# Attention into experts: side work of the first expert tiles spread over tiles 1 to 6

## The reference

```
f = 1/(1+exp(-f_logit))
state = f[t]*state + outer(k[t], v[t]);  y[t] = q[t] @ state
logits = x @ w_gate + modality_bias[modality_id];  e = argmax(logits)
out[mask] = softmax(logits)[e] * (relu(x[mask] @ w1[e]) @ w2[e])      # experts, F=1024
xn = x/rms(x)*rms_g
y = (silu(xn @ w_gate) * (xn @ w_val)) @ w_out                        # dense layer, F=1536
```

## Time and profile before

| | us |
|---|---|
| runs | 873.43, 869.73, 873.39 (median 873.39) |
| profiled execution, its own time | 871.66 |
| its span in the profile | 869.9 |
| TensorE busy | 835.2 |
| VectorE, ScalarE, GpSimd busy | 470.8, 389.7, 167.0 |
| mean granted clock of TensorE | 0.983 |

### The profile page before, as it was taken

One profiled execution on the slowest core, in us unless ns is written; L12 is line 12 of the kernel. 1 busy time (PEld: TensorE's weight loads), 2 busy tenths in 40 slices (PEclk: granted clock), 3 DMA queues, 4 the chain that ended last, 5 costly groups with the idle time before them and its releaser, 6 DMA issues.

```text
span 869.9 us, 15469 instructions
## 1 busy us (share of the span) xinstructions
PE 835.2 (96%) x5332; PEld 763.1 (88%) x5332; DVE 470.8 (54%) x773; ACT 389.7 (45%) x750; POOL 167.0 (19%) x165
## 2 busy tenths in 40 slices
PE   6999999779999999989999999999999999999997
PEld 6788888779999999989888888888888888888886
DVE  7799998687666666653444343334333333433332
ACT  5788886375666555653322321331242133123112
POOL 5335352408654000000000100110010010001001
PEclk8899999889999999999999999999999999999999
DMA  9767766398988797750200200100020000000000
GB/s 186 159 141 165 172 147 216 139 371 256 294 257 264 245 348 241 267 146 20 73 1 1 73 0 1 64 9 0 0 72 0 0 27 9 0 0 36 0 0 36
DMA packets 44082, 96.49 MB, mean 111 GB/s; under 512 B 9168, under 2 KB 25040, under 8 KB 43920
## 3 DMA queue, kind: packets, MB, share of 16 engines
q1 hardware_dynamic: 39952, 85.81, 33.5%
q0 software_dynamic: 3840, 9.47, 3.0%
q10 hardware_dynamic: 256, 0.79, 0.4%
HBM read 76.75 MB, written 19.29 MB: 110 GB/s over the span
## 4 chain that ended last, share of the span: by engine, by line
PE 77%; issue 1%; DVE 1%; ACT 1%; POOL 0%; DVEq 0%; ACTq 0%
PE h_ps L1778 16%; PE h_ps L1780 15%; PE h_ps L1779 15%; PE ym_ps L1778 7%; PE ym_ps L1780 7%; PE ym_ps L1779 7%; PE xTm_ps L1778 3%; PE xTm_ps L1779 3%; PE xTm_ps L1780 3%; PE xT_ps L1795 1%; PE xTm_ps L1786 1%; POOL out L1442 0%; DVE h_lo L1690 0%; DVE w_lo L1663 0%; ACT w_hi L1460 0%
## 5 line engine op out<-in xcount | busy, mean ns | idle before, releaser
L1753 DVE TENSOR_TENSOR gs<-h_ps,sig 128x512 f32<-128x512 f32 x72 | 49.8, 692 | 178.1 <-ACT sig L1554 178.1
L1554 ACT ACTIVATE sig<-h_ps 128x512 f32<-128x512 f32 x72 | 43.1, 598 | 171.6 <-PE h_ps L1780 171.6
L1565 ACT CAST h_hi<-hid 128x512 fp32r<-128x512 f32 x72 | 44.6, 620 | 150.3 <-DVE hid L1756 150.3
L1778 PE MATMUL h_ps<-x_hi,w_hi 128*128 128x256 f32 x312 | 89.6, 287 | 7.7 <-DVEq L1681 5.1
L1780 PE MATMUL h_ps<-x_lo,w_hi 128*128 128x256 f32 x312 | 89.3, 286 | 0.0
L1779 PE MATMUL h_ps<-x_hi,w_lo 128*128 128x256 f32 x312 | 89.1, 285 | 0.0
L1778 PE MATMUL h_ps<-w_hi,wg_hi 128*128 128x512 f32 x216 | 85.7, 397 | 0.0
L1780 PE MATMUL h_ps<-w_lo,wg_hi 128*128 128x512 f32 x216 | 84.7, 392 | 0.0
L1780 PE MATMUL h_ps<-w_lo,wv_hi 128*128 128x512 f32 x216 | 84.2, 390 | 0.0
L1778 PE MATMUL h_ps<-w_hi,wv_hi 128*128 128x512 f32 x216 | 84.0, 389 | 0.0
L1779 PE MATMUL h_ps<-w_hi,wv_lo 128*128 128x512 f32 x216 | 84.0, 389 | 0.0
(11 more groups left out here) (222 smaller groups left out, 1899.6 us busy)
## 6 DMA issues: line engine op xcount, KB each, us to landing
w_raw<-in_w SPq DMA_DIRECT2D x52, 384.0 KB, 5.1
w_in<-in_w SPq DMA_DIRECT2D x52, 384.0 KB, 5.2
qkf_in<-in_qkf SPq DMA_DIRECT2D x43, 288.0 KB, 4.8
y_sorted<-x_group SPq DMA_DIRECT2D x13, 384.0 KB, 3.4
v_in<-in_v SPq DMA_DIRECT2D x24, 192.0 KB, 4.0
x_regions<-zero_row SPq DMA_DIRECT2D x12, 384.0 KB
x_group<-x_regions SPq DMA_DIRECT2D x12, 384.0 KB, 4.1
g_in<-in_wg SPq DMA_DIRECT2D x3, 768.0 KB, 7.3
```

Of the source, the lines that this page charges most:

```text
L1554: nc.scalar.activation(sig[:], g_ps, ACT.Sigmoid).then_inc(sig_done, 1)
L1565: nc.scalar.copy(h2_hi[:, fb % 2], hid[:]).then_inc(h2_hi_done, 1)
L1753: nc.vector.tensor_tensor(gs[:], g_ps, sig[:], ALU.mult).then_inc(gs_done, 1)
L1778: nc.tensor.matmul(out, hi, rhs_hi, start=first, stop=False)
```

## The change

In the attention's last steps the last tile's keys are no longer turned or copied (they would only feed a state that nobody reads); its reading goes to the bank `ks_ps` that this leaves free, ahead of the rows of the tile before. ScalarE's w1 casts move, and `lo_w1(3)` goes from there into the experts. SyncE loads the first expert's weights ahead of the last two v tiles. In tile 0 ScalarE makes all four w2 casts at once, the count of the last chunk stands in the middle of `hidden(0)`, and the thirds, the scores, exp, table load, token rows and gates leave for the loop: third i to the end of tile i+1, exp and table load to tile 2, token rows to tile 2, gates to tile 3. The by_token writes come 8 each behind thirds 3, 4 and 5; the load of w_out moves from tile 7 to 8.

```
@@ attention, SyncE, then ScalarE
             first.load_weights(sp, e, w1, w2, ahead_sems)
+            for b in range(2):
+                load_v(*tile(CH, b, 2))
-                if t := tile(c, b, 1):
+                if (t := tile(c, b, 1)) and not at(c, CH):      # the copy of turned keys
+                if at(c, CH) and b == 1:
+                    first.hi_w1(nc, act, 3, ahead_sems)
+                    kept(tile(c, b, 2), ks_ps)
...
@@ attention, VectorE and TensorE
-                    first.lo_x(nc, dve, xT_ps, ahead_sems)
-                    first.lo_w1(nc, dve, 3, ahead_sems)
+                if at(c, CH) and b == 2:
+                    first.lo_x(nc, dve, xT_ps, ahead_sems)      # ahead of logits
+                if at(c, CH) and b == 1:
+                    pe.wait_ge(ks_done, NT - 1)
+                    read(c, b, tile(c, b, 2), ks_ps)
...
@@ experts, SyncE
+            for g in range(GR):
+                sp.sem_inc(w2_landed[g], 16)                    # ahead of the two thirds
...
@@ experts, GpSimd
-            pool.wait_ge(pos_ready, 1)
-            pool.wait_ge(gate_ready, 1)
+                if i == KD:
+                    pool.wait_ge(pos_ready, 1)
+                    pool.wait_ge(gate_ready, 1)
...
@@ experts, ScalarE
-            hi_w2(0, 0)
+            for g in range(GR):
+                hi_w2(0, g)
                 hi_h(1)
-                if place == "first":
-                    hi_w2(0, 2)
-                    act.wait_ge(shifted, 1)
-                    nc.scalar.activation(prob, biased, ACT.Exp).then_inc(exp_ready, 1)
-                    nc.scalar.preload_act_table_set("sigmoid_and_others")
-                    hi_w2(0, 3)
...
                 if place == "first":
-                    hi_third(0)
...
-                    with act.If(j < 2 * KD):
-                        for i in range(EARLY, 2 * KD):
-                            with only(act, j, i - 1):
+                    with act.If(j < 2 * KD + 1):
+                        for i in range(2 * KD):
+                            with only(act, j, i + 1):
                                 hi_third(i)
+                                if i == 1:
+                                    act.wait_ge(shifted, 1)
+                                    nc.scalar.activation(prob, biased, ACT.Exp).then_inc(exp_ready, 1)
+                                    nc.scalar.preload_act_table_set("sigmoid_and_others")
@@ experts, VectorE
-            dve.sem_inc(w1_split, GR)
+            dve.sem_inc(w1_split, GR - 1)
             rt.choose(nc, dve, CH - 1, marks, 0)
+            lo_w1(0, GR - 1)
             lo_w2(0, 0)
...
                 if place == "first":
-                    rows_of_tokens()
-                    gates_of_tokens()
+                    rows_of_tiles()
+                if place == "middle":
+                    with dve.If(j < 4):
+                        with only(dve, j, 1):
+                            shifted_scores()
+                        with only(dve, j, 2):
+                            rows_of_tokens()
+                        with only(dve, j, 3):
+                            gates_of_tokens()
```

## The result

Four executions of the changed kernel gave 884.7 to 889.3 us, median 886.88; four of the kernel before 868.9 to 873.43, median 871.56. The ratio is 1.019, with a 95% interval of 1.0165 to 1.0216: slower, inside the range, and 0.9 us from the predicted 886. The profiled execution took 888.39 us (span 886.6), 16.7 us more than that of the kernel before.

The account below looks back on a forecast made before the run. PE, busy 835.2 of 869.9 us, was taken as the bound, so only its stops or slowing count. Terms -0.85, -5.5, +13.8, +1.3 and +5.0 sum to +13.75 us: 885.4 on 871.66, stated as 886, range 878 to 892.

Parts of the forecast that it names:

- end of attention: Barrier between attention and experts: four transposes off the last scatter's chain end it earlier, -0.85 us, bounds nothing and 2.7.
- tiles 0 and 1: First two expert tiles: waits shrink or go and the half clock goes, -5.5 us, bounds 1 and 9.
- waits behind thirds: Loop tiles after thirds 0 to 5: table loads delay `h_lo`, so PE waits before `gather_y(0)`, +13.8 us.
- load in the last tile: Last expert tile: a whole table load ahead of the first square delays `h_hi(0)`, +1.3 us, bounds 0 and 1.3.
- clock: Behind five new PE waits: two in three halve the clock at 1.5 us each, +5.0 us, bounds 0 and 7.5.
- The step that decided: Loop: two loads on ScalarE's chain, less 0.27 us slack, make PE wait 2.5 us behind each of four thirds.
- One sign: Loop turns with two loads: PE waits 2.5 us before `gather_y(0)`, named in the profile as waiting for `h_lo`.
- third 1's tile: Tile after third 1: exp, its table load and the head's load make PE wait 2.8 us.
- rival D: Tiles 0 to 3: early gains fail through a held DVE instruction or late rows and w2; 890 us, chance 0.12.
- A: Loop's table loads: reloading the set already in is nearly free, so not slower; 869.1 us, chance 0.07.
- B: Loop's table loads: they are hidden, leaving only the gains, -6.35 us; 865.3 us, chance 0.04.
- C: Table loads: each costs twice its length since what follows must start afresh; 901 us, chance 0.03.

Follow-up runs that it names:

- after_again: The changed kernel run once more without alteration, on chip C: 885.54 us, ratio 1.0177 to the kernel before.

## Why the prediction was right

The terms of the sum, on the profiled executions:

| term | predicted | measured |
|---|---|---|
| end of attention | -0.85 | -0.74 (163.09 to 162.35; 0.6 from the count on) |
| tiles 0 and 1 | -5.5 | -4.95 |
| waits behind thirds | +13.8 | +15.9 |
| load in the last tile | +1.3 | 0 |
| clock | +5.0 | +6.5 |
| sum | +13.75 | +16.7 |

**The loop.** The step that decided held within 0.06 us in the ordinary tiles: 2.5 us predicted behind thirds 2 to 5, 2.45, 2.45, 2.45 and 2.54 measured; tiles behind no third kept 17.64 us. All of it was read from one chain and a slack of 0.27 us. The loads themselves, 21 in all with the one ahead of attention, each take 1283 ns. One sign came otherwise: these waits are not named as waiting for `h_lo` but as `issue`. In tile 5 `h_lo` ended at 278.59 and PE started at 278.69, so it was `h_lo` all the same.

**The same step failed in one tile.** I put third 1's tile at 2.8 us, of loads and exp. It was 4.96, and 4.95 without any load. I had counted the token rows of VectorE as moved into a tile with room, and not looked at what stands right behind them (`h_lo(0)`) and beside them (GpSimd's split of the third that ScalarE has just cast). The hold on VectorE that I feared elsewhere (rival D) fell on them. ScalarE's relu, behind exp and both loads, ended 1.8 us ahead of the rows (232.65 us), so the later one alone counts:

```profile
230.24 0.60 ACT L1494 ACTIVATE h_hi<-h_ps 128x512 fp32r<-128x512 f32 x1
```

By my estimate from these rows ScalarE alone would have made PE wait 2.7 us, close to the 2.8 predicted. Had I priced the rows at 2.7 us with the 0.60 us of the loop's head, I would have seen 1.9 us even without GpSimd, and hidden behind the loads.

**The end of attention.** VectorE's last instruction ended at 157.71 in place of 160.50, 2.8 us earlier, and GpSimd's last scatter was issued at 157.04 in place of 157.59:

```profile
157.04 0.97 POOL L136 DMA_INDIRECT x_regions<-x_group,row  x1 [0.30 <-issue]
157.53 0.18 DVE L652 TENSOR_REDUCE logits<-x_ps 128x8 f32<-128x32 f32 x1
```

The experts' start moved with the scatter, 0.6 us from the count on, as the step had it. But PE's wait there grew to 5.69 us, where I had written 4.2 as a sign: PE was done with attention 1.4 us earlier and waited for the same scatter.

**Tiles 0 and 1.** The rows of tile 1 were what is late next, as said: 2.54 us at `turn_x`, then 0.84 for `x_lo`. The wait in tile 1 was 0.93 for 0.95 predicted, and no half clock came behind either. The gain was 0.55 us smaller.

**The clock.** Of the waits of 2.45 to 2.54 us one of four was followed by the half level, where I had said two of three. The price was off the other way: behind the wait of 4.96 us the clock stayed at half for 5.6 us, tile 3 lost 25.60 - 17.64 - 4.96 = 3.0 us and tile 4 21.80 - 17.64 - 2.45 = 1.7, and after the loop's exit, where the kernel before had kept its clock, 0.41 of 4.21 us were lost, 1.7. The profile of after_again (885.68 us) has the same waits and half levels in the loop and at its exit, and takes 243.94 us from the experts' first matmul to the exit against 243.84. The 2.7 us between the two executions lie ahead of the experts (159.55 and 162.35), in code that is the same: from 20 to 40 us the granted clock was 1.00 in the one and 0.88 in the other. A difference of 3 us in the total can come from there alone.

```profile
234.04:239.60 5.56, 5.56 (x20) 5.56 (x21) 2.71 (x4) 0.83 (x1) 0.00 (x0) 0.50 0.81 277
278.69:281.70 3.01, 3.01 (x19) 3.01 (x20) 3.01 (x3) 1.76 (x3) 2.62 (x2) 1.00 0.97 284
```

**The last tile.** No wait of 0.25 us stands there, yet the load was not free on ScalarE's side:

```profile
407.23 1.28 ACT L1092 ACT_TABLE_LOAD   x1 [2.42 <-issue]
412.40 0.41 PE L1788 MATMUL ym_ps<-w_hi,h_hi 128*128 128x384 f32 x1 [0.15 <-issue]
```

It began behind the same idle time as the square before, and `h_lo(0)` ended 6.10 us behind the loop's exit in place of 4.78, 1.3 later. PE, at the half clock, was ready for its gather only at 6.06 us behind the exit, 1.5 us later than before. So the whole load that I had counted was there, and hid behind a fall of the clock; the two don't add up here.

**Rivals.** A and B are out by the two runs with loads added. C (a load costs twice its length) is out by each pair in the fence of tile 5, where the next instruction starts 0.01 to 0.02 us behind the load's end. The drain that the Trainium skill gives beside the load for a switch to a different set ("ScalarE: Activation LUTs", "What ACT_TABLE_LOAD costs") shows in none of the runs. That the total came so near is in part luck: four errors (+2.2 for the rows, +0.7 for the early gains, +1.5 for the clock, -1.3 for the last tile) left 3 us, and the median of the executions lay 1.5 us under the profiled one. The mechanism of the loop is not luck: the loads alone, added to the kernel before, cost 13.2 us.

## What to carry to other kernels

A preload of an activation table inside a branch or a loop makes the table's state uncertain at every point where paths meet, and the build pays for that with loads at the loop's head; count the loads in the built instruction order, or keep exp in the table that is in and switch outside the loop. Moving work off a crowded engine to a tile "with room" is priced by what stands directly behind it and by what the engine beside it does then: the same instructions cost 0 us ahead of a wait that exists anyway, 1.9 us ahead of a tight hand-over, and 5.0 us there beside GpSimd's elementwise work. Long rows of small indirect writes were beside stops of all compute engines on one chip, and lots of four, tried on another chip, were not; that short lots cure it is not shown. A variant is best timed on more than one chip before it is believed, and a profiled total is best split at a common point, here the experts' first matmul, before it is compared.

## What the runs showed of the hardware

- A table load of the set that is in costs the full 1283 ns.
- VectorE instructions of 0.24 to 0.36 us took 1.20 to 1.36 us beside a GpSimd elementwise subtraction in three pieces (3.74 us), one hold for each; those behind its end took 0.18 to 0.49 us, about as without it.
- With 8 or 24 indirect writes in a row, the compute engines stood still for 0.4 to 13.7 us on one of three chips (A). With 24 in a row on chip B and with 8 on chip C no such stop was seen. What passes between GpSimd's writes and the other engines there is open.
- The kernel before ran alike on all three chips (medians 869.67 to 871.72).
